# The 64-token tile of each expert in the second mixture: high and low parts in one stationary operand

## The reference

```python
order = np.argsort(-flat)                 # all (token, expert) logits, largest first
for idx in order:                         # an expert takes at most cap = N // E = 576 tokens
    tok, e = idx // E, idx % E
    if assigned[tok] >= 0 or counts[e] >= cap: continue
    assigned[tok] = e; counts[e] += 1
for e in range(E):
    h = np.maximum(x[assigned == e] @ w1[e], 0.0)    # 512 -> 1024
    out[assigned == e] = h @ w2[e]                   # 1024 -> 512
```

## Time and profile before

| | |
|---|---|
| runs (3): median, lowest, highest | 1489.16, 1486.3, 1492.13 us |
| profiled execution: time, span | 1488.37 us, 1486.6 us |
| TensorE busy | 1317.2 us (89%), mean granted clock 0.941 |
| VectorE busy | 939.4 us (63%) |
| ScalarE, GpSimd busy | 444.3 us (30%), 398.9 us (27%) |
| chain that ended last, TensorE's L719 | 52% of the span |

### The profile page before, as it was taken

The page is one execution under the profiler, slowest core; times in us unless marked ns, Lnnn a source line. Parts: engine busy times, 40 slices in busy tenths (PEclk is TensorE's granted clock), DMA queues, the critical chain, the costliest instruction groups (busy, mean ns, idle before and its releaser), DMA issues.

```text
span 1486.6 us, 23689 instructions
## 1 busy us (share of the span) xinstructions
PE 1317.2 (89%) x8032; PEld 1053.5 (71%) x8032; DVE 939.4 (63%) x2238; ACT 444.3 (30%) x785; POOL 398.9 (27%) x323
## 2 busy tenths in 40 slices
PE   5988717897999999999995279999999999999997
PEld 5877616786888888888884156777677677777885
DVE  1566794677577776776676757676566656675520
ACT  1555521222222222222220112323232223323431
POOL 1244425757515271570000010202020111111210
PEclk9899958999999999999997579999999999999999
DMA  9999127695415153351100313131313131413100
GB/s 230 259 236 308 57 53 283 213 358 176 143 44 156 44 157 93 107 156 44 44 29 15 113 36 121 54 128 50 132 44 138 45 139 36 146 36 138 51 32 18
DMA packets 71155, 173.27 MB, mean 117 GB/s; under 512 B 11624, under 2 KB 30136, under 8 KB 70400
## 3 DMA queue, kind: packets, MB, share of 16 engines
q1 hardware_dynamic: 46576, 108.61, 24.0%
q0 software_dynamic: 12368, 40.92, 8.8%
q10 hardware_dynamic: 12096, 22.19, 4.7%
HBM read 130.47 MB, written 41.23 MB: 115 GB/s over the span
## 4 chain that ended last, share of the span: by engine, by line
PE 67%; DVE 12%; DMA 7%; issue 6%; POOL 6%; ACT 1%; SPq 1%; POOLq 0%; DVEq 0%; ACTq 0%
PE bank L719 52%; PE bank L762 4%; POOL w_lo L557 3%; DMA xst<-x_rows,tok_i 2%; PE bank L818 2%; PE o_ps L681 2%; PE bank L755 2%; DVE cmp L1298 1%; DMA x_sorted<-xst 1%; DMA v_sb<-in_v 1%; POOL xrow L565 1%; DVE ohb L1388 1%; DMA w_sb<-in_moe_w 1%; POOL w_hi L555 1%; PE bank L748 1%
## 5 line engine op out<-in xcount | busy, mean ns | idle before, releaser
L1280 DVE SCALAR_TENSOR_TENSOR bank<-bank,factor,wg2b 128x512 f32<-128x512 f32 x336 | 254.6, 758 | 10.4
L1267 DVE TENSOR_TENSOR hT_lo<-bank,hT_hi 128x512 fp32r<-128x512 f32 x166 | 106.7, 684 | 184.9 <-ACT hT_hi L1008 184.8
L719 PE MATMUL bank<-w_hi,xT_hi 128*128 (+1 forms) x664 | 199.2, 417 | 12.5 <-POOL w_lo L557 7.7
L975 ACT ACTIVATE h<-bank 128x512 f32<-128x512 f32 x166 | 99.3, 598 | 356.7 <-PE bank L719 356.7
L719 PE MATMUL bank<-w_lo,xT_hi 128*128 (+1 forms) x664 | 192.7, 407 | 0.0
L611 POOL DMA_INDIRECT xg<-y_rows,gat_i x40 | 45.6, 1140 | 545.2 <-DVE sca_i L1398 400.5
L719 PE MATMUL bank<-w_hi,xT_lo 128*128 (+1 forms) x664 | 187.6, 403 | 0.0
L719 PE MATMUL bank<-w_hi,hT_hi 128*128 (+1 forms) x664 | 180.8, 412 | 6.2 <-DVE score L1283 3.9
L719 PE MATMUL bank<-w_hi,hT_lo 128*128 (+1 forms) x664 | 175.7, 400 | 0.0
L719 PE MATMUL bank<-w_lo,hT_hi 128*128 (+1 forms) x664 | 173.6, 399 | 0.0
L719 PEld LDWEIGHTS bank<-w_hi,xT_lo 128*128 128x128 f32 x664 | 125.8, 191 | 30.0
(11 more groups left out here) (243 smaller groups left out, 1677.5 us busy)
## 6 DMA issues: line engine op xcount, KB each, us to landing
w_sb<-in_moe_w SPq DMA_DIRECT2D x112, 512.0 KB, 6.3
y_rows<-y ACTq DMA_DIRECT2D x43, 256.0 KB, 3.0
x_sorted<-xst SPq DMA_DIRECT2D x41, 260.0 KB, 5.6
xg<-x_sorted ACTq DMA_DIRECT2D x41, 260.0 KB, 2.8
k_sb<-in_k SPq DMA_DIRECT2D x16, 576.0 KB, 12.0
v_sb<-in_v SPq DMA_DIRECT2D x16, 576.0 KB, 14.9
q_sb<-in_q SPq DMA_DIRECT2D x8, 1152.0 KB, 17.7
x_rows<-xrow POOLq DMA_DIRECT2D x16, 576.0 KB, 6.7
```

The costliest lines, as they stand in the source:

```text
L719: mm = pe.matmul(ps, a[:, i % chunks, :], b[:, i % chunks, cols], start=(i == 0), stop=(i == 3 * chunks - 1))
L975: act.activation(h[:, half * HALF:(half + 1) * HALF], h_ps[half][:, :], ACT.Relu).then_inc(s_h, 1)
L1267: dve.tensor_tensor(hT_lo[:, half * 4:(half + 1) * 4, :].rearrange("p a b -> p (a b)"), th_ps[half][:, :], hT_hi[:, half * 4:(half + 1) * ...
L1280: ch.link(dve.scalar_tensor_tensor(out=prod_ps[:, :], in0=y1_ps[t % 2][:, :], scalar=factor[:, t:t + 1], in1=wg2b[:, e, :], op0=ALU.mult, ...
```

## The change

**The short tile.** For the tile of 64 tokens a chunk of `xT_hi` and `hT_hi` holds the high parts in columns 0 to 63 and the low parts in columns 64 to 127. One matmul with all 128 columns against the high weights gives high x high in PSUM rows 0 to 63 and low x high in rows 64 to 127; one with columns 0 to 63 against the low weights adds high x low to the lower rows. So a product is 2 x chunks matmuls in place of 3 x chunks (`short_in_parts`). The two halves of the rows have to be added: behind the first layer this happens while `h` is turned, by a plain float32 matmul with `fold` (two 64x64 identities, one above the other) in place of a transposition, with the relu moved behind it; behind the second layer ScalarE copies rows 64 to 127 out (`upper_y`) and VectorE adds them to rows 0 to 63 (`halves_added`, duty y). Before its first matmul `short_in_parts` waits for the low part of its activations, which `in_parts` waits for ahead of the third pass.

**The points.** A tile's points follow from its matmuls; a phase has 112 instead of 120. `WHERE` and `FIRST` are set anew: the steps of a search (0 to 26) stood in the cycle at 56, 59, 62, 66, 69, 72, 77, 80, 83, 92, 95, 98, 103, 106, 109, 114, 117, 0, 5, 8, 11, 16, 19, 22, 27, 30, 35 and stand at 49, 52, 55, 59, 62, 65, 70, 73, 76, 84, 87, 90, 94, 97, 100, 104, 107, 110, 2, 5, 8, 12, 15, 18, 21, 24, 29. In a phase the first layers of the tiles start at points 0, 20, 44, 68, 92 and the second layers behind them at 12, 32, 56, 80, 100 (before: 0, 24, ... and 12, 36, ...). Duty h3 moves from behind step 6 to behind step 7, h0 from 18 to 19, h1 from 24 to 25 with y0 ahead of it, h4 from 12 to 13. The list's pieces L1388 move to steps 5, 6 and 7. `weights_high` takes all eight pieces in the last three tiles of the phase before.

```diff
-    PER_TILE = 24
-    cycle = PER_TILE * T2
+    FULL, SHORT = 6, 4
+    FIRST_AT, SECOND_AT, cycle = [], [], 0
+    for g in range(T2):
+        FIRST_AT.append(cycle)
+        cycle += 2 * (SHORT if g == T2 - 1 else FULL)
+        SECOND_AT.append(cycle)
+        cycle += 2 * (SHORT if g == 0 else FULL)
-    def timed(start, rounds, spread, behind):
+    def timed(start, rounds, behind):
-            at += [start + spread * i for i in range(3)]
+            at += [start, start + 3, start + 6]
-    WHERE = timed(-64, (10, 11, 15, 11, 11, 11, 11, 11), 3, (0, 3, 8, 13))
-    FIRST = [None] * (LISTED + 1) + [1] + timed(6, (8, 8, 8, 8), 3, (1, 4, 9, 13))
+    WHERE = timed(-63, (10, 11, 14, 10, 10, 10, 10, 9), (0, 3, 8, 14))
+    FIRST = [None] * (LISTED + 1) + [1] + timed(6, (7, 7, 8, 8), (0, 3, 7, 11))
...
+    windows = []
-        for kind, due, need in (("h", PER_TILE * g + 3, PER_TILE * g + 19), ("x", PER_TILE * g + 15, PER_TILE * g + 27)):
-            at, n = min((x + c, n) for n, x in enumerate(WHERE) for c in (0, cycle) if x + c >= due)
+        follows = (FIRST_AT + [cycle])[g + 1]
+        windows.append(("h", g, FIRST_AT[g] + 3, SECOND_AT[g] + (-1 if g == 0 else 7)))
+        if g == 0:
+            windows.append(("y", g, follows + 3, SECOND_AT[1] - 2))
+        windows.append(("x", g, SECOND_AT[g] + 3, follows + (-1 if g == T2 - 2 else 3)))
+    for kind, g, due, need in windows:
+        at, n = min((x + c, n) for n, x in enumerate(WHERE) for c in (0, cycle) if x + c >= due)
+        assert at <= need
+        DUTIES[n].append((kind, g))
+        if at < WHERE[0] + cycle and kind + str(g) not in ("h0", "y0"):
+            at, n = min((x, n) for n, x in enumerate(FIRST) if x is not None and x >= due)
-            DUTIES[n].append((kind, g))
-            if at < WHERE[0] + cycle and (kind, g) != ("h", 0):
-                at, n = min((x, n) for n, x in enumerate(FIRST) if x is not None and x >= due)
-                assert at <= need
-                FIRST_DUTIES[n].append((kind, g))
+            FIRST_DUTIES[n].append((kind, g))
-    LOW_BESIDE = {11: (0,), 12: (1,), 13: (2,), 14: (3,), 19: (4,), 20: (5,), 22: (6,), 23: (7,)}
+    LOW_BESIDE = {12: (0,), 13: (1,), 14: (2,), 15: (3,), 19: (4,), 20: (5,), 22: (6,), 23: (7,)}
...
+        fold = sb("fold", [P, LAST])
...
+        upper = xst[0][0:LAST, 0:DM]
...
-            def first_in_parts(n, w, half, low_w, point):
+            def short_in_parts(ps, act, w, cols, chunks, high_w, low_w, low_x, done, point):
+                pe.wait_ge(*low_x)
+                if high_w is not None:
+                    pe.wait_ge(s_whi, high_w)
+                if low_w is not None:
+                    pe.wait_ge(s_wlo, low_w)
+                order = [(0, P), *((c, LAST) for c in range(chunks)), *((c, P) for c in range(1, chunks))]
+                for i, (c, rows) in enumerate(order):
+                    mm = pe.matmul(ps[0:rows, :], act[:, c, 0:rows], w[rows < P][:, c, cols],
+                                   start=(i == 0), stop=(i == 2 * chunks - 1))
+                    if i == 2 * chunks - 1:
+                        mm.then_inc(done, 1)
+                    if i % 2 == 1:
+                        point(i // 2)
+            def first_in_parts(n, w, half, low_w, point, short=False):
+                if short:
+                    short_in_parts(h_ps[half][:, :], xT_hi, w, slice(half * HALF, (half + 1) * HALF), KC,
+                                   None, None, (s_xlo, n + 1), s_l1, point)
+                    return
-            def second_in_parts(n, w, high_w, low_w, point):
+            def second_in_parts(n, w, high_w, low_w, point, short=False):
+                if short:
+                    pe.wait_ge(s_y, n)
+                    short_in_parts(y_ps[:, :], hT_hi, w, slice(0, DM), FC, high_w, low_w, (s_hlo, n * 2 + 2), s_l2, point)
+                    return
...
+                rows = LAST if vv == T2 - 1 else P
+                if rows < P:
+                    alone(pe)
-                    mm = pe.transpose(tx_ps[:, c * P:(c + 1) * P], xgs[w % 2][:, c:DM:KC], ident[:, :])
+                    mm = pe.transpose(tx_ps[:, c * P:c * P + rows], xgs[w % 2][0:rows, c:DM:KC], ident[0:rows, 0:rows])
-            def h_turned(n):
+            def h_turned(n, short=False):
+                        if short:
+                            mm = pe.matmul(th_ps[half][:, i * P:i * P + LAST], h[:, half * 4 + i:F:FC], fold[:, :], start=True, stop=True)
+                            continue
...
+                    short = vv == T2 - 1
-                    first_in_parts(n, w1_parts, 0, low, lambda i: searches(kk, PER_TILE * vv + i))
-                    first_in_parts(n, w1_parts, 1, None, lambda i: searches(kk, PER_TILE * vv + 6 + i))
+                    for half in range(2):
+                        at = FIRST_AT[vv] + half * (SHORT if short else FULL)
+                        first_in_parts(n, w1_parts, half, low if half == 0 else None, lambda i: searches(kk, at + i), short)
-                                        lambda i: searches(kk, PER_TILE * vv + 12 + i))
+                                        lambda i: searches(kk, SECOND_AT[vv] + i), vv == 0)
-                        for i in range(PER_TILE // 2):
-                            searches(kk, PER_TILE * vv + 12 + i)
-                    h_turned(n)
+                        for i in range(2 * SHORT):
+                            searches(kk, SECOND_AT[vv] + i)
+                    h_turned(n, short)
...
-            def relu(n):
+            def relu(n, short=False):
-                    act.activation(h[:, half * HALF:(half + 1) * HALF], h_ps[half][:, :], ACT.Relu).then_inc(s_h, 1)
+                    act.activation(h[:, half * HALF:(half + 1) * HALF], h_ps[half][:, :], ACT.Copy if short else ACT.Relu).then_inc(s_h, 1)
...
-            def rows_high(n):
+            def rows_high(n, short=False):
+                if short:
+                    act.activation(xT_hi[:, :, 0:LAST], tx_ps[:, :].rearrange("p (c t) -> p c t", t=P)[:, :, 0:LAST], ACT.Copy).then_inc(s_xT, 1)
+                    return
...
-            def hT_high(n):
+            def upper_y(j, u):
+                w = u * T2 + T2 - 1
+                act.wait_ge(s_l2, j * (2 * T2) + (T1 + w + 2))
+                act.wait_ge(s_y, j * (2 * T2) + (T1 + w))
+                act.activation(upper, y_ps[LAST:2 * LAST, :], ACT.Copy).then_inc(s_yu, 1)
+            def hT_high(n, short=False):
+                    if short:
+                        act.activation(hT_hi[:, half * 4:(half + 1) * 4, 0:LAST],
+                                       th_ps[half][:, :].rearrange("p (c t) -> p c t", t=P)[:, :, 0:LAST], ACT.Relu).then_inc(s_hT, 1)
+                        continue
...
-                    relu(n)
+                    short = vv == T2 - 1
+                    relu(n, short)
-                        rows_high(n + 1)
-                    if vv == 0:
-                        weights_high(kk, u, (6, 7))
+                        rows_high(n + 1, vv == T2 - 2)
-                        y_copy(j - 1 + u, 1 - u, T2 - 1)
-                    hT_high(n)
+                        upper_y(j - 1 + u, 1 - u)
+                    hT_high(n, short)
-                        weights_high(kk + 1, 1 - u, ((0, 1), (2, 3), (4, 5))[vv - (T2 - 3)])
+                        weights_high(kk + 1, 1 - u, ((0, 1, 2), (3, 4, 5), (6, 7))[vv - (T2 - 3)])
...
-            weights_high(0, 0, range(PIECES // 2 + 2))
+            weights_high(0, 0, range(PIECES))
...
-            def rows_low(n):
+            def rows_low(n, short=False):
+                if short:
+                    dve.tensor_tensor(xT_hi[:, :, LAST:2 * LAST], tx_ps[:, :].rearrange("p (c t) -> p c t", t=P)[:, :, 0:LAST],
+                                      xT_hi[:, :, 0:LAST].bitcast(F32), ALU.subtract).then_inc(s_xlo, 1)
+                    return
-            def hT_low(n):
+            def hT_low(n, short=False):
+                    if short:
+                        four = slice(half * 4, (half + 1) * 4)
+                        dve.scalar_tensor_tensor(out=hT_hi[:, four, LAST:2 * LAST], in0=th_ps[half][:, :].rearrange("p (c t) -> p c t", t=P)[:, :, 0:LAST],
+                                                 scalar=0.0, in1=hT_hi[:, four, 0:LAST].bitcast(F32),
+                                                 op0=ALU.max, op1=ALU.subtract).then_inc(s_hlo, 1)
+                        continue
+            def halves_added(kk, u):
+                w = u * T2 + T2 - 1
+                dve.wait_ge(s_yu, kk + 1)
+                dve.wait_ge(s_out[w % 2], (kk - u) // 2 * T2 * 16 + w // 2 * 16 if isinstance(kk, int) else (kk * T2 + (T2 - 1 - w % 2)) * 8)
+                dve.tensor_tensor(ys[w % 2][0:LAST, :], y_ps[0:LAST, :], upper, ALU.add).then_inc(s_y, 1)
...
-                        hT_low(T1 + tile - 1)
+                        hT_low(T1 + tile - 1, g == 0)
-                        rows_low(T1 + tile + 1)
```

(28 more changed lines are left out.)

## The result

| | before | after |
|---|---|---|
| median of 8 runs each | 1488.54 us (1485.01 to 1492.21) | 1497.05 us (1493.12 to 1498.97) |
| ratio | | 1.0053, 95% interval 1.0035 to 1.0070 |
| profiled execution, span | 1488.37, 1486.6 us | 1497.26, 1495.1 us |

The change makes the kernel slower by half a per cent. The forecast was 1479 us and a range of 1466 to 1490.

What follows compares the result with a forecast made beforehand. TensorE's matmuls were taken to bound the kernel, with waits on VectorE's search steps where it idles. Terms summed to -14.8 us, -10.3 with the clock's +4.5: 1478.1 us against the profiled execution, 1479 against the median, range 1466 to 1490.

Steps and rivals of the forecast that it cites:

- 128 matmuls: Short tiles' two layers: 16 matmuls fewer in each of 8 phases, at 0.233 us each, -29.8 us.
- fold: Short tiles' turning of h: 8 float32 products replace 8 transpositions, 0.95 us more per phase, +7.6 us (+1.0 to +12.5).
- clock: TensorE's clock falls behind half of the six new waits at search step 8, +4.5 us (bounds 0 and 9).
- rows of 64: Short tile's gather and transpositions with half the columns: nothing to -1 us, taken as 0.
- steps 6 to 8: Search steps beside the list's work: TensorE waits 2.0 us where 1.1 stood, in six phases, +5.4 us.
- TIES: Search's tie step: y0 and h1 now delay VectorE's answer, a wait of about 0.2 us in six phases, +1.2 us.
- loop turns (VectorE's): Where VectorE's program turns its loop: one point less for TensorE lengthens the wait by 0.5 us, two turns, +1.0 us.
- phase 0: Search in an empty second layer: one compare step less saves 2.3 us, 1.4 us of matmul saving lost, -1.0 us.
- end: Last second layer waits for the low part (0.15 us), output passes ScalarE then VectorE (0.65 more), +0.8 us.
- fourth rival: Fold: a plain product costs four transpositions, 19.4 us in all instead of 7.6, 1491 us; chance 0.05.
- slower rival: Search steps 13 to 16: VectorE late again, 1.5 us wait plus 1.5 clock fall in six phases, 1501 us; chance 0.07.
- last rival: Short tile's matmuls: the second and third passes cost what they did, near 1504 us; chance 0.03.

Runs made afterwards that it cites:

- w = 1 or 2: Changed kernel with ScalarE writing the short tile's h so the fold reads neighbouring (1) or every second column (2): 1473.67 us and, one run, 1477.4 us.
- w = 4 or 8: Fold reading every fourth column of h (4), against the changed kernel, which reads every eighth (8): 1492.25 us in one run, and 1497.05 us.
- experiment 2: Changed kernel, but ScalarE writes the short tile's h so that the fold reads neighbouring columns: 1473.67 us, 0.9879 of the kernel before.
- experiment 5: Kernel before, three passes and 120 points kept, with only the change's closer search steps and side work placement: 1491.71 us, ratio 1.0012.
- second kernel: The kernel of experiment 2: changed kernel with the fold reading neighbouring columns of h, 1473.67 us.

## Why the prediction was wrong

By its own steps, forecast and measured (us; "pair" is the two profiles from the first TIES on):

| step | forecast | measured | from |
|---|---|---|---|
| 128 matmuls | -29.8 | -29.8 | eight in 1.85 us, also with 64 stationary columns |
| fold | +7.6 | +22.4 | 8 x (3.61 - 0.81) |
| clock | +4.5 behind step 8 | 0 there, +7.2 behind five folds | the matmuls behind each take 1.4 to 1.5 us more |
| rows of 64 | 0 | +2 | 0.62 and a gap of 0.1 ahead, against 0.39 for full rows |
| steps 6 to 8 | +5.4 | +3.2 | 1.50 in place of 0.96, six times |
| TIES | +1.2 | 0 | no wait in these phases |
| loop turns (VectorE's) | +1.0 | +0.9 | 2.69 and 2.53 us, as against the earlier trace rows |
| phase 0 | -1.0 | -1.5 | 63.8 us from TIES to TIES for 66.7, then a wait of 3.55 for 2.15 |
| end | +0.8 | +3 | below |
| TensorE's loop turn | not a term | -1.8 | the wait below is gone |
| sum | -10.3 | +5.6 | pair: +2.9 |

The row that the forecast did not have is a wait in the kernel before, at the place where TensorE's program turns its loop:

```profile
1183.28 0.73 PE L719 MATMUL bank<-w_hi,xT_hi 128*128 128x512 f32 x2 [1.78 <-ACT w_hi L1015]
```

Behind a fast fold (w = 1 or 2) or plain transpositions an idle time of 0.7 to 1.9 us stands at this place, and behind each of the slow folds (w = 4 or 8) none: the slow fold covers it.

The sum of the single readings still misses the pair by 2.7 us. In phases 2 to 6 they come out 0.5 to 0.8 us too high each. In phase 2, where the clock fell in neither profile (TIES to TIES 76.5 us before, 76.1 after), the readings give +0.1 and the trace -0.4: the transpositions of the full tiles take 0.4 us less there in all, which I had not read.

**The fold failed, as a size:** +7.6 us were forecast, +22.4 measured, and the 3.61 us of a group are over the 2.4 that the prediction named as a sign of being wrong. The step said: "The third is nearest; since a transposition of the same block costs 0.101, I take 0.11". 0.11 is right for a block of neighbouring columns (0.106 in experiment 2), but the fold reads every eighth column of h, and there a record of the plain float32 product takes 0.226, twice as much. All of the earlier trace rows read neighbouring columns, while the row that I leaned on for the step, the transposition of h in the earlier trace rows, reads the very same columns at 0.101, less than the plain product takes with neighbouring ones. So the nearest row by shape was not the nearest by access. Even the upper end (0.148, +12.5 us) lay under the truth.

**The rule of the Trainium skill** that stood against the edit ("TensorE: Matmul & The Clock Gate", section "Terms": the transpose mode is four times faster for FP32) came nearer than the rows that I set against it. The fourth rival made the fold 3.2 us in a phase and gave 1491 us; measured are 3.6 us and 1497. With every eighth column the eight products take 4.5 times the 0.81 us of the transpositions, near the rule. But the rule alone does not explain it: with neighbouring columns the same eight take 1.70 us, 2.1 times and not four times the transpositions.

**The clock** is the second step that failed, by its place. The step put half of six falls behind the wait at step 8. Behind that wait of 1.4 to 1.5 us it never fell, neither here nor in the other five kernels that have it (36 waits). It fell behind 3.6 us of slow weight loads, in which TensorE shows no idle time, five times of seven. That the forecast's +4.5 lies not far from the +7.2 of these falls is an accident.

**The search** went nearly as worked out. The waits at step 8, at the loop turns and at the start of search 2 came within 0.3 us of the forecast. At steps 6 and 7 the forecast was too dark by 0.35 and 0.2 us: VectorE starts L1474 before ind has quite ended and L1540 without the gap of 0.2 us, and L869 to L873 leaves it 2.0 us. The closer steps cost no more than the longer gaps would have: experiment 5. The +5.4 was too large by these two waits, and it set 1.1 us from a single phase against the new ones where the average before was 0.96.

**Phase 0** is right in part by luck. Behind its waits near 876 us the clock fell for 6.8 us in the profile before and not in the changed kernel's. Of the eight kernels with the short tile's new points, four have 63.6 to 63.8 us from TIES to TIES, without such a fall, and four 65.8 to 66.9, with one. With a fall on both sides the -1.5 would be +0.5 to +1.6.

**The end** was worked out too small: the last second layer waits 1.02 us for the low part (0.78 for the high part before), and behind this wait its next 8 matmuls take 3.38 us instead of 1.85, at the slow clock again. The clock fell there in four of the eight kernels with the short tile. The lines are TensorE's and VectorE's:

```profile
1474.19 3.79 PE L811 MATMUL bank<-fold,h 128*128 128x64 f32 x16
...
1478.43 0.42 DVE L1341 SCALAR_TENSOR_TENSOR hT_hi<-bank,hT_hi 128x256 fp32r<-128x256 f32 x1 [1.48 <-ACT hT_hi L1073]
1479.00 0.54 PE L756 MATMUL bank<-w_hi,hT_hi 128*128 128x512 f32 x1 [1.02 <-DVE hT_hi L1341]
1479.34 3.55 PE L756 MATMUL bank<-w_lo,hT_hi 128*64 128x512 f32 x8
1482.72 1.80 PE L756 MATMUL bank<-w_hi,hT_hi 128*128 128x512 f32 x7
```

**The slower rival**, a second late step at 13 to 16, did not come: no wait stands there. The verdict is slower all the same, through a term of my sum and not through a rival of that sign. The last rival, that the passes cost what they did, did not come either: eight matmuls with 64 stationary columns took 1.85 us. Its price of 1504 us left out the clock term of the forecast's own sum; with it, it is 1509.

**What stays open.** The medians differ by 8.5 us, the pair from the first TIES on by 2.9. Whether the attention's part (224.2 to 230.6 us over ten executions) is chance alone, or whether the clock fell more often in the other runs of the changed kernel, a profile of one execution doesn't tell.

## What to carry to other kernels

A price from a nearby row holds only if the row reads its operands in the same way: before a transposition is replaced by a product, look at the step between its stationary columns, and if it is 16 bytes or more, let the engine that writes the tile lay it out for the product. The rows of the profile, a fold of 3.6 us where 1.8 was expected, show such a thing at once, and a change whose main saving is right should then be mended and not dropped: with the layout and one duty moved, this one is 1.7% faster than before.

## What the runs showed of the hardware

- A plain float32 product with a 128x128 stationary block takes 0.106 us a record with neighbouring columns, 0.112 with every second, 0.221 with every fourth and 0.226 with every eighth; a transposition of the block with every eighth column takes 0.101.
- TensorE's granted clock fell from 2.4 to 1.2 GHz at the end of, or just behind, 3.5 to 3.6 us of float32 products at 0.22 us a record without idle time, in 11 of the 21 places with large matmuls behind them, and stayed at 2.4 GHz behind 36 waits of 1.4 to 1.5 us between large matmuls. It fell behind an idle time of 1.29 us in the second kernel, and not behind one of 2.71 us there, so that the length of a wait alone does not decide it.
- ScalarE writes a 128x512 tile from PSUM in 0.60 us in order, in 0.60 and 0.65 with four and two neighbours together, and in 1.12 us where each element goes 512 bytes from the last.
- Turning 64 rows took TensorE 0.62 us, turning 128 rows 0.39; a separate instruction stood ahead of the 64 rows.
